# The second feed-forward block by Strassen's scheme: seven half-block products in six of nine token groups

## The reference, cut to what matters

```python
x = attention(q, k, v)                      # (2304, 512)
c = softmax(x @ phi)                        # (2304, 32)
x = c @ slot_out                            # (2304, 512)
h = np.maximum(x @ w_in, 0.0)               # (2304, 2048)
out = h * h @ w_out                         # (2304, 512)
```

## Time and profile before

| | us |
|---|---|
| median of 3 runs (lowest, highest) | 424.74 (424.46, 425.55) |
| the profiled execution, its own time | 423.91 |
| its span (first to last instruction) | 422.1 |
| PE busy in the span | 402.9 |
| DVE busy | 243.4 |
| ACT busy | 218.8 |
| one group of 256 tokens in the last block | 23.84 |

### The profile page before, as it was taken

How to read it: one execution, slowest core, us unless ns; L and a number is a source line. 1 busy time by engine, 2 the same in 40 slices (tenths; PEclk the granted TensorE clock), 3 DMA queues, 4 the chain that set the end, 5 groups by cost and what they waited for, 6 DMA issues and landing times.

```text
span 422.1 us, 7944 instructions
## 1 busy us (share of the span) xinstructions
PE 402.9 (95%) x2873; PEld 310.1 (73%) x2873; DVE 243.4 (58%) x680; ACT 218.8 (52%) x560; POOL 97.9 (23%) x94
## 2 busy tenths in 40 slices
PE   6699999999989999989899999999999999999996
PEld 5588888888777554333688888888888888888884
DVE  4788888888855543113999545454545445454520
ACT  3889898989854311003965444444443434444420
POOL 4578787878650010000142000000000000000000
PEclk9999999999999999999999999999999999999999
DMA  6689898997725799999600101010101001010101
GB/s 183 160 238 291 246 309 257 289 269 237 201 79 178 251 371 398 405 383 386 222 2 0 51 0 51 0 50 2 50 2 50 0 0 50 0 50 2 50 0 50
DMA packets 49858, 61.34 MB, mean 145 GB/s; under 512 B 25504, under 2 KB 33696, under 8 KB 48288
## 3 DMA queue, kind: packets, MB, share of 16 engines
q1 hardware_dynamic: 49280, 60.37, 42.7%
q10 hardware_dynamic: 544, 0.52, 0.4%
HBM read 56.16 MB, written 4.72 MB: 144 GB/s over the span
## 4 chain that ended last, share of the span: by engine, by line
PE 84%; ACT 5%; DMA 4%; DVE 4%; SPq 1%; issue 1%; POOL 0%; ACTq 0%; POOLq 0%
PE psum L1319 15%; PE psum L1320 15%; PE psum L1321 15%; PE psum L1033 6%; PE psum L1077 6%; PE psum L1059 5%; PE psum L1300 4%; DMA win_sb<-in_moe_w_in 3%; PE psum L1227 3%; ACT probs L831 3%; PE psum L992 2%; PE psum L1248 2%; PE psum L1137 2%; PE psum L1042 2%; PE psum L1014 2%; SPq L447 1%
## 5 line engine op out<-in xcount | busy, mean ns | idle before, releaser
L1319 PE MATMUL psum<-wout_hi,act_hi 128*128 128x512 f32 x288 | 113.2, 393 | 1.8 <-DVE wout_lo L755 1.5
L1320 PE MATMUL psum<-wout_lo,act_hi 128*128 128x512 f32 x288 | 112.9, 392 | 0.0
L1321 PE MATMUL psum<-wout_hi,act_lo 128*128 128x512 f32 x288 | 112.1, 389 | 0.0
L781 DVE TENSOR_TENSOR sq_h<-relu_h 128x512 f32<-128x512 f32 x72 | 56.3, 782 | 78.4 <-ACT relu_h L940 78.3
L940 ACT ACTIVATE relu_h<-psum 128x512 f32<-128x512 f32 x72 | 43.1, 599 | 92.0 <-PE psum L1300 86.1
L831 ACT ACTIVATE probs<-probs,row_min 128x256 f32<-128x256 f32 (+1 forms) x128 | 60.1, 471 | 13.5 <-DVE row_min L562 13.5
L503 POOL TENSOR_TENSOR probs<-probs,row_inv 128x1024 f32<-128x1024 f32 x31 | 59.2, 1928 | 23.2 <-DVE row_inv L613 23.2
L1321 PEld LDWEIGHTS psum<-wout_hi,act_lo 128*128 128x128 f32 x288 | 54.1, 188 | 11.8
L1319 PEld LDWEIGHTS psum<-wout_hi,act_hi 128*128 128x128 f32 x288 | 54.1, 188 | 11.8 <-issue 1.9
L1320 PEld LDWEIGHTS psum<-wout_lo,act_hi 128*128 128x128 f32 x288 | 54.3, 189 | 8.7
L785 DVE TENSOR_TENSOR act_lo<-sq_h,act_hi 128x512 fp32r<-128x512 f32 x72 | 49.8, 692 | 5.4 <-ACT act_hi L943 0.6
(11 more groups left out here) (143 smaller groups left out, 436.1 us busy)
## 6 DMA issues: line engine op xcount, KB each, us to landing
ring<-in_moe_w SPq DMA_DIRECT2D x16, 1024.0 KB, 6.2
ring<-in_moe_w SPq DMA_DIRECT2D x4, 2048.0 KB, 13.6
out_x<-out_sb SPq DMA_DIRECT2D x9, 512.0 KB, 2.8
q_raw<-in_q SPq DMA_DIRECT2D x16, 256.0 KB, 3.6
v_in<-in_v SPq DMA_DIRECT2D x32, 128.0 KB, 2.6
ring_late<-in_moe_w SPq DMA_DIRECT2D x2, 2048.0 KB, 9.4
ring_x<-in_moe_w SPq DMA_DIRECT2D x2, 2048.0 KB, 8.0
win_sb<-in_moe_w_in SPq DMA_DIRECT2D x4, 1024.0 KB, 14.4
```

The costliest lines, as they stand in the source:

```text
L781: nc.vector.tensor_tensor(sq_h[:, u % 2, :], relu_h[:, u % 2, :], relu_h[:, u % 2, :], ALU.mult).then_inc(sq_done, 1)
L1319: mm(to, hi, wout_hi[:, c, :], start=first_of, stop=False)
L1320: mm(to, hi, wout_lo[:, c, :], start=False, stop=False)
L1321: last = mm(to, lo, wout_hi[:, c, :], start=False, stop=last_of)
```

## The change

Groups 0 to 2 keep the old products (`CONV = 3`). Groups 3 to 8 treat the 256 tokens as two halves, the 2048 hidden units as two halves (`KH = 8` chunks each) and the 512 output columns as two halves (`NH = 256`). The 2 x 2 block product is formed from seven block products (`PRODUCTS`) in place of eight, each with the three-matmul split, and all with 256 columns. The order within a step is `FIRST_ORDER`, or `LAST_ORDER` in a group's last step; accumulators are half banks (`acc`).

A group has four steps (`NB = 4`) of two chunk pairs (i = 0, 1). For a step:

- PE, `hidden_steps`: four 256-column matmuls into banks 0 and 1 (two per i), always these two banks.
- ACT, `next_steps`: first the float32r copies of the step before (`high_steps`: two of 896 elements per partition, seven operands of 128), then two ReLUs of 512 and one square of 1024 in place.
- DVE, `next_steps`: first the differences of the step before (`low_steps`: two of 896), then the sums S3 (256 elements), S1 and S2 in one (512), S4 (256).
- PE, `products`: 7 products x 2 chunks x 3 matmuls of 256 columns.

At a group's end ACT copies products 1 and 4 out (256 elements each), and DVE combines the seven in six instructions (five of 256 elements, one of 512) in `take_out`; the last group is stored in two halves. The four sums of weight blocks (`T1` to `T4`) are formed, rounded and split in groups 1 and 2, by tables of places: `T_OF_DVE` (8 `form_t` and 8 `low_t`, 1024 elements each) and `T_OF_ACT` (8 `high_t`). For unit 12 on (`SQ_OF_DVE`) the plain groups compute the float32 square on ACT (ReLU, square, copy) and not on DVE. `act_hi` and `act_lo` become five rotating slots (`conv`). The hardware loop now holds groups 4 to 7.

The core of the diff (PE's products and its order within a group, ACT's work for a step and DVE's sums):

```diff
+            def hidden_steps(n, j):
+                for i in range(2):
+                    pe.wait_ge(relu_done, FU * n + 2 * j + i - 1)
+                    for k in range(2):
+                        at = P * (KH * k + 2 * j + i)
+                        last = mm(psum[:, i, FT * k:FT * k + FT], mix[:, at:at + P], cols, start=True, stop=True)
+                    last.then_inc(l1_done, 1)
...
-                        mm(to, hi, wout_hi[:, c, :], start=first_of, stop=False)
-                        mm(to, hi, wout_lo[:, c, :], start=False, stop=False)
-                        last = mm(to, lo, wout_hi[:, c, :], start=False, stop=last_of)
...
+                mm(to, hi, w_hi, start=clears, stop=False, skip_group_check=True)
+                mm(to, hi, w_lo, start=False, stop=False, skip_group_check=True)
+                return mm(to, lo, w_hi, start=False, stop=c == KH - 1, skip_group_check=True)
...
+            def strassen(n, par):
+                for j in range(NB):
+                    if j == 0:
+                        hidden_steps(n, NB - 1)
+                    elif not is_last(n):
+                        hidden_steps(n + 1, j - 1)
...
+            def high_steps(n, j):
+                act.wait_ge(sums_done, NB * (n - CONV) + j + 1)
+                for i in range(2):
+                    nc.scalar.copy(step_hi[j][:, i, :, :], step_raw[j][:, i, 1:8, :]).then_inc(hi_done, 1)
+
+            def next_steps(n, j):
+
+                if j > 0:
+                    high_steps(n, j - 1)
+                elif not isinstance(n, int) or n > CONV:
+                    high_steps(n - 1, NB - 1)
...
+                    act.wait_ge(l2_used, NB * n + j + L2_AT - NB)
...
+                for i in range(2):
+                    act.wait_ge(l1_done, FU * n + 2 * j + i + 1)
+                    nc.scalar.activation(step_raw[j][:, i, 0:4, :],
+                                         psum[:, i, :].rearrange("p (s x) -> p s x", x=P), ACT.Relu).then_inc(relu_done, 1)
+                act.wait_ge(relu_done, FU * n + 2 * j + 2)
+                sq = step_raw[j][:, :, 0:4, :]
+                nc.scalar.activation(sq, sq, ACT.Square).then_inc(sqA_done, 1)
...
+            def sums(n, j):
+                a = step_raw[j]
+                dve.wait_ge(sqA_done, NB * n + j + SQ_ACT_AT)
+                nc.vector.tensor_tensor(a[:, :, S3, :], a[:, :, A21, :], a[:, :, A11, :], ALU.subtract
+                                        ).then_inc(s3_done, 1)
+                dve.wait_ge(s3_done, NB * (n - CONV) + j + 1)
+                nc.vector.tensor_tensor(a[:, :, S1:S2 + 1, :], a[:, :, A21:S3 + 1:S3 - A21, :],
+                                        a[:, :, A22:A22 + 1, :].to_broadcast([P, 2, 2, P]), ALU.add).then_inc(s12_done, 1)
+                dve.wait_ge(s12_done, NB * (n - CONV) + j + 1)
+                nc.vector.tensor_tensor(a[:, :, S4, :], a[:, :, A12, :], a[:, :, S2, :], ALU.subtract
+                                        ).then_inc(sums_done, 1)
...
+FIRST_ORDER, LAST_ORDER = (6, 5, 7, 3, 1, 2, 4), (1, 2, 4, 6, 5, 7, 3)
+AHEAD_STEPS = {4: 0, 5: 1, 6: None, 7: 2}
```

More of the change, by code:

```diff
@@ L40 @@
 AHEAD = 4
+CONV = 3
+KH, NH = FC // 2, DM // 2
+NB = KH // 2
+A21, A11, A22, A12, S1, S2, S3, S4 = range(8)
+T1, T3, T2, T4 = range(4)
 XSLOTS = 11
@@ L315, in last_block, with is_last @@
             step(2, 0)
-            with eng.Fori(1, (NFT - 3) // 2) as n2:
+            step(3, 1)
+            with eng.Fori(CONV // 2 + 1, (NFT - 1) // 2) as n2:
+                step(n2 * 2, 0)
                 step(n2 * 2 + 1, 1)
-                step(n2 * 2 + 2, 0)
-            step(NFT - 2, 1)
             step(NFT - 1, 0)
+        def is_last(n):
+            return isinstance(n, int) and n == NFT - 1
         ROUNDS = [(0, 1), (2, 3)]
@@ new lines, in low_t, with low_steps @@
+            def low_t(half, t):
+                cs = slice(4 * half, 4 * half + 4)
+                dve.wait_ge(t_high, 4 * half + t + 1)
+                nc.vector.tensor_tensor(t_lo[:, t, cs, :], t_sum[:, t, cs, :], t_hi[:, t, cs, :].bitcast(F32),
+                                        ALU.subtract).then_inc(t_ready, 1)
+            def low_steps(n, j, only=(0, 1)):
+                for i in only:
+                    dve.wait_ge(hi_done, FU * n + 2 * j + i + 1)
+                    nc.vector.tensor_tensor(step_lo[j][:, i, 1:8, :], step_raw[j][:, i, 1:8, :],
+                                            step_hi[j][:, i, :, :].bitcast(F32), ALU.subtract
+                                            ).then_inc(lo_done, 1)
@@ new lines, in products @@
+            def products(n, par, j, xs):
+                pe.wait_ge(lo_done, FU * n + 2 * j + 2)
+                if isinstance(n, int) and n == CONV and j % 2 == 0:
+                    pe.wait_ge(t_ready, 2 * j + 4)
+                for x in xs:
+                    if j == 0:
+                        wait_bank(n, par, x)
+                    for c in (2 * j, 2 * j + 1):
+                        last = product(n, par, x, c)
+                    if j == NB - 1 and x in (4, 5):
+                        last.then_inc(p_done, 1)
+                return last
@@ new lines, in last_products @@
+            def last_products(n, par):
+                pe.wait_ge(lo_done, FU * n + KH)
+                for x in LAST_ORDER:
+                    if x == 3:
+                        wait_bank(n, par, x)
+                    for c in range(0 if x == 3 else KH // 2, KH):
+                        last = product(n, par, x, c)
+                    if x in (4, 5, 7):
+                        last.then_inc(p_done, 1)
+                last.then_inc(l2_used, 1)
+            def strassen(n, par):
+                for j in range(NB):
+                    if j == 0:
+                        hidden_steps(n, NB - 1)
+                    elif not is_last(n):
+                        hidden_steps(n + 1, j - 1)
+                    if is_last(n) and j == NB // 2:
+                        last_products(n, par)
+                        return
+                    xs = LAST_ORDER if j == NB - 1 else FIRST_ORDER
+                    products(n, par, j, [x for x in xs if x != 3] if is_last(n) else xs).then_inc(l2_used, 1)
@@ L1364, in step @@
                     return
+                if not isinstance(n, int) or n >= CONV:
+                    strassen(n, par)
+                    return
                 for u in range(FU):
```

334 lines of the change are left out of this document (263 added, 71 removed).

## The result

The changed kernel takes 421.08 us (median of 4 runs, 420.75 to 421.3), beside 424.6 (423.71 to 425.55) for the kernel before: ratio 0.9908, 95% interval 0.9882 to 0.9935. The forecast was 421.6. The profiled execution took 421.05 us with a span of 419.3 (the time from its first to its last instruction); 420.8 was forecast for it.

The account below looks back on a forecast made before the run. PE's matmuls bound the old kernel; afterwards an ACT-DVE ring would. Start at 264.5, 23 rings (129.5) and five group ends (4.0), then the tail and smaller store gave 420.8 profiled, plus 0.83: 421.6 us, 8-in-10 range 412 to 429.

Parts of the forecast that it names:

- The ring: Groups 3 to 8: ACT and DVE wait on each other in each step, 5.58 us against PE's 5.27.
- The hardware loop: Steps in the loop: register instructions add nothing to 0.13 us a ring; half taken, giving 5.65.
- the slow-loop rival: Waits in the hardware loop cost 0.11 us at each hand-over, making the kernel slower, 429 us; chance 0.18.
- The end of a group: DVE's six combining instructions delay the next sums by 0.8 us, five times, 4.0 in all; bounds nothing and 1.3.
- The start: ACT's first ReLU of group 3's first step, placed at 264.5 us in the profile.
- The last difference: DVE's last difference of group 8's last step, placed at 404.8 us, before PE's last products.
- PE's step: One step on PE in groups 3 to 8: 46 matmuls of 256 columns at 0.1146 us, 5.27 us.
- The PE-bound rival: Groups 3 to 8: the ring is under 5.27 us and PE stays the bound, 407.3 us; chance 0.13.
- The last store: Program's end: 256 KB store in place of 512, 0.66 us less; other half's store leaving earlier, 0.6 more.
- Groups 1 and 2: Work added to ACT and DVE there fits under PE's time and costs nothing.
- Weight loads: Rival: loads bind in long rows of 256-column matmuls, doubling each to 0.229 us, 535 us in all; chance 0.02.
- The signs: Profile after: groups of 23.4 us, PE idle 0.3 a step, ACT idle 1.6 before copies, group-end steps 0.8 longer.

Follow-up runs that it names:

- experiment 1: Changed kernel with ACT's copies of the step before moved behind the square, and DVE's sums ahead of those differences: 411.22 us, ratio 0.9652.
- 6: On experiment 1's order, buffers of steps 1 and 3 moved from 96 to 32 modulo 128 bytes: 412.67 us, ratio 0.9714.
- 7: On experiment 1's order, weights and buffers of steps 0 and 2 moved from 32 to 96 modulo 128 bytes: 413.36 us, ratio 0.9763.
- 8: On experiment 1's order plus 22 warm-up transposes on PE, step_hi of steps 0 and 2 moved from 32 to 96 modulo 128: 408.95 us, ratio 0.9599.
- experiment 4: Changed kernel with the last four of DVE's six group-end instructions moved behind the next group's first step: 419.36 us, ratio 0.9844.

## Why the prediction was right

The main step held: PE's cut matmuls don't set the time; a ring of ACT and DVE does. By its steps:

- **The ring**: 5.58 forecast, 5.53 measured. Its parts by the rows of ACT and DVE above: copies 1.70 (forecast 1.65), ReLUs 1.10 (1.13), square with its hand-over 1.09 (1.08), the sums with theirs 0.45, 0.73 and 0.46 (0.465, 0.73, 0.525). The interpolated sizes were 940 ns for 925, 1061 for 1040, 1088 for 1090 and, for 256 elements on DVE, 0.42 to 0.43 us for 0.425. The hand-over from DVE to ACT is what came out smaller, 0.03 and not the 0.10 of the earlier trace rows.
- **The hardware loop**: 0.065 a ring forecast, nothing measured (5.53 in both places). The register instructions run while the engine is idle, as the argument against the slow-loop rival said. With the ring's size that is 2.3 us less over 23 rings than forecast.
- **The end of a group**: 0.8 forecast, 0.76 measured at the first and 0.84 to 1.07 at the others, 4.4 for five instead of 4.0.
- **The start**: ACT's first ReLU of a step stands at 265.59 and not 264.5. 1.0 of this is the block's late start under the lower clock, which the forecast could not know from one profile. The ring's first turn took 6.15, 0.6 more than the others; the forecast had none of it. In it ACT's ReLU waits 0.50 us for a plain product of group 2 (L1546):

```profile
271.74 1.09 ACT L1142 ACTIVATE step_raw<-psum 128x512 f32<-128x512 f32 x2 [0.50 <-PE psum L1546]
```

- **The last difference** ends at 404.73; 404.8 was forecast. The errors cancel: 1.1 + 0.6 + 0.4 late, 2.3 early, and 0.1 late in the last turn. That the sum is right to 0.1 is luck; that no part is off by more than 2.3 us is not.
- **PE's step, the mis-sized term**: 5.27 forecast, from 0.1146 for a 256-column matmul, which was half of a 512-column one. In long rows they are 0.118 to 0.120 apart: from 278.75 to 283.78 there are 42 in 5.03 us. A step is thus 5.45 to 5.52, within 0.1 of the ring. The PE-bound rival had 407.3; experiment 1, where PE is the bound, takes 411.2. The ring hid this but for the last products: 11.6 us from 404.79 to DVE's last piece, 0.4 more than the forecast.
- **The last store**: 0.8 measured. The forecast names two gains, 0.66 and 0.6, but its "together 3.1" is 2.5 with only one of them; with both it would have been 3.7, and the profiled execution 420.2 for 421.05.
- **The median**: the forecast adds 0.83 to the profiled execution, as before. Here the median stands 0.03 above it. So 421.6 is 0.5 too much though 420.8 was 0.25 too little, which is luck again.
- **Groups 1 and 2** cost nothing, as said: PE enters the first step of group 3 at 277.92, 1.95 later than before and 1.5 later than the forecast's 276.4, of which 1.0 is the late start, 0.46 the four more hidden matmuls and 0.29 a wait for ACT; 0.2 is not placed:

```profile
277.92 0.99 PE L1556 MATMUL psum<-combT,mix 128*128 128x256 f32 x4 [0.29 <-ACT step_raw L1142]
```

- **Weight loads** did not bind: PEld is busy 22.07 us of 22.88 while PE runs. The Trainium skill ("TensorE: Matmul & The Clock Gate", What overlaps and what doesn't) has such loads overlap only between different row groups; the trace still does not agree, now over rows of 42 with new weights for each.
- **The signs**: ACT's idle stretch of 1.68 ahead of the copies (1.6 forecast) and the group's end came as said. A group is 22.97 to 23.20, not 23.4. PE's idle 0.3 us a step ahead of the hidden matmuls is not in the profile: it shows a wait there once a group, 0.29 to 0.66 us. That follows from the mis-sized matmul, and by this sign alone the PE-bound rival could not have been told from the ring.

What it comes to: 2.75 us a group were to be cut from PE (2.0 at the spacing measured), and with the ring and the group's end 0.6 to 0.9 of them reached the time: ACT's copies past a group's end stand 22.97 to 23.20 apart (309.55, 332.52, 355.72, 378.70, 401.67), for 23.84. Six groups would make about 5 us. The last products, which come late, took one of them, and the later start of group 3 two; the smaller last store added 0.8, which comes to about the 2.9 by which the profiled executions differ. Experiment 1 gives most of the difference back.

## What to carry to other kernels

When a change takes work from a full engine and hands it to two half-empty ones that pass a step back and forth, add their turn up as a chain, with each hand-over: here two engines at 74% and 69% of a group made a bound that no busy share shows. Then look for the order in which each has something of another step to do while the other computes; that edit was worth 9.9 us here (some 2.3 of them by the closer spacing of PE's matmuls that came with it), nearly three times what the whole change had brought. Where two bounds lie within 0.1 us of each other, the busy share does not tell them apart, but an added link on one side and less work on the other do. And price a matmul from a long row of the very shape; halving a wider one was 3 to 5% short in the changed kernel.

## What was not expected of the hardware

- The spacing of 256-column matmuls with new float32r weights depends on where the two operands lie in a partition: 0.1133 us or 0.118 to 0.120, by their places modulo 128 bytes (experiments 1, 6, 7, 8). With the places unchanged it also differs between two orders of ACT's and DVE's work (0.1178 in the changed kernel, 0.1133 in experiment 1), so the rule is not complete.
- After equal waits of 3.0 us for a transfer the granted clock stayed at 1.00 in one execution and fell to 0.50 in the profiled execution of another kernel with the same instructions there; after 2.65 us it stayed at 1.00 in the changed kernel, and after 2.68 it was 0.50 in experiment 4. Executions of the kernel before with a lower mean clock have spans that are 1 to 4 us longer.
- From DVE's last sum to ACT's copies the hand-over is 0.03 us (302.80 + 0.43 to 303.26), where the earlier trace rows have 0.10 from DVE to ACT behind an instruction of 2.89.
